# Gate products moved behind the first unit's transposes and first layer, expert 0's second-layer weights issued one step earlier, first rows rounded without a wait

## The reference

```python
def _moe_ref(x, w_in, w_out):
    h = x @ w_in
    g = h - np.tanh(h)
    return (g @ w_out).astype(np.float32)

def _moe2_ref(x, expert_emb, tau, w1, w2):          # x: 3072 x 384, 8 experts, width 1024
    xn = x / (np.linalg.norm(x, axis=-1, keepdims=True) + 1e-06)
    en = expert_emb / (np.linalg.norm(expert_emb, axis=-1, keepdims=True) + 1e-06)
    logits = xn @ en.T / tau
    expert_idx = np.argmax(logits, axis=1)
    logits_shift = logits - logits.max(-1, keepdims=True)
    probs = np.exp(logits_shift)
    probs /= probs.sum(-1, keepdims=True) + 1e-09
    gate_w = probs[np.arange(N), expert_idx]
    ...
    for e in range(E):
        mask = expert_idx == e
        ...
        h = np.maximum(x[mask] @ w1[e], 0.0)
        out[mask] = gate_w[mask, None] * (h @ w2[e])
```

## Time and profile before

| | |
|---|---|
| median of 3 runs | 851.17 us (847.74 to 852.49) |
| the profiled execution | 848.86 us, span 847.1 us |
| mean granted TensorE clock | 0.982 |
| TensorE busy | 819.8 us (97%) |
| VectorE, ScalarE, GpSimd busy | 640.3, 507.1, 217.9 us |
| moved by the transfers | 157.89 MB, mean 186 GB/s |

### The profile page before, as it was taken

One profiled execution on the slowest core, in us unless ns is written; L12 is line 12 of the kernel. 1 busy time (PEld: TensorE's weight loads), 2 busy tenths in 40 slices (PEclk: granted clock), 3 DMA queues, 4 the chain that ended last, 5 costly groups with the idle time before them and its releaser, 6 DMA issues. The chain is left out here.

```text
span 847.1 us, 18162 instructions
## 1 busy us (share of the span) xinstructions
PE 819.8 (97%) x5844; PEld 745.2 (88%) x5845; DVE 640.3 (76%) x983; ACT 507.1 (60%) x1057; POOL 217.9 (26%) x239
## 2 busy tenths in 40 slices
PE   8999989999999999999999999789999999999995
PEld 7767768889999999999999998689999999999994
DVE  8979959999998998998998997714546363637552
ACT  5756777767667667667667765215546363636552
POOL 6345524321111111111112331122222223132111
PEclk9999999999999999999999999769999999999998
DMA  9989943225234234224223755479696859693540
GB/s 245 279 255 278 297 131 94 66 80 179 100 106 154 87 109 151 99 87 161 101 100 123 235 188 182 172 244 387 240 332 238 292 203 388 245 362 121 176 160 9
DMA packets 86430, 157.89 MB, mean 186 GB/s; under 512 B 8060, under 2 KB 23566, under 8 KB 86385
## 3 DMA queue, kind: packets, MB, share of 16 engines
q1 hardware_dynamic: 58672, 100.82, 36.5%
q10 hardware_dynamic: 23744, 45.69, 15.0%
q0 software_dynamic: 3968, 10.82, 3.6%
HBM read 117.97 MB, written 40.70 MB: 187 GB/s over the span
## 5 line engine op out<-in xcount | busy, mean ns | idle before, releaser
L1303 POOL TENSOR_TENSOR ew_l<-ew_raw,ew_h 128x512 fp32r<-128x512 f32 x48 | 62.3, 1299 | 272.3 <-DVE poly L1521 268.0
L1227 PE MATMUL y_ps<-wout_h,g_h 128*128 128x392 f32 x384 | 130.8, 341 | 0.4 <-DVE g_l L1512 0.4
L1228 PE MATMUL y_ps<-wout_l,g_h 128*128 128x392 f32 x384 | 130.4, 340 | 0.0
L1229 PE MATMUL y_ps<-wout_h,g_l 128*128 128x392 f32 x384 | 130.3, 339 | 0.0
L1227 PE MATMUL h_ps<-xT_h,win 128*128 (+1 forms) x288 | 113.3, 394 | 1.2 <-DVE diff L1502 0.8
L1229 PE MATMUL h_ps<-xT_h,win 128*128 (+1 forms) x288 | 113.3, 394 | 0.0
L1228 PE MATMUL h_ps<-xT_l,win 128*128 (+1 forms) x288 | 112.8, 392 | 0.0
L1698 DVE SCALAR_TENSOR_TENSOR ex_hT_l<-e_bank,ex_hT_h 128x512 fp32r<-128x512 f32 x48 | 33.2, 691 | 102.8 <-ACT ex_hT_h L1952 88.0
L1853 PE MATMUL e_bank<-ex_xT_h,w_ex 128*128 128x256 f32 x288 | 81.8, 284 | 3.5 <-DVE ex_xT_l L1691 2.9
L1521 DVE COPY_PREDICATED poly<-large,diff 128x512 f32<-128x512 uint8 x96 | 72.0, 750 | 17.5 <-DVE poly L1517 17.5
L1854 PE MATMUL e_bank<-ex_xT_l,w_ex 128*128 128x256 f32 x288 | 81.5, 283 | 0.0
(11 more groups left out here) (244 smaller groups left out, 1994.0 us busy)
## 6 DMA issues: line engine op xcount, KB each, us to landing
w_raw<-in_w ACTq DMA_DIRECT2D x26, 1536.0 KB
ew_raw<-in_w SPq DMA_DIRECT2D x48, 256.0 KB, 2.7
w_h<-ew_h SPq DMA_DIRECT2D x48, 256.0 KB, 2.3
w_l<-ew_l SPq DMA_DIRECT2D x48, 256.0 KB, 2.0
w_ex<-w_h SPq DMA_DIRECT2D x8, 1536.0 KB
w_ex<-w_l SPq DMA_DIRECT2D x8, 1536.0 KB
kv_sb<-in_kv SPq DMA_DIRECT2D x24, 384.0 KB, 5.6
krT_sb<-in_krT SPq DMA_DIRECT2D x44, 192.0 KB, 6.1
```

The source lines that it names most:

```text
L1227: pe.matmul(out, lh, rh, start=start, stop=False)
L1228: pe.matmul(out, lh, rl, start=False, stop=False)
L1229: return pe.matmul(out, ll, rh, start=False, stop=stop)
L1303: pool.tensor_tensor(ew_l[:, slot, :], raw, ew_h[:, slot, :].bitcast(F32), ALU.subtract).then_inc(ew_l_made, 1)
```

## The change

Five edits, all at the boundary of the two blocks.

1. The buffer that holds the experts' weights is laid out anew (`unit_weights`, `second_weights`, `raw_at`; WIDE is 3072 values per partition). Both slots of second-layer weights now lie together at 2 to 6 WIDE, and the first-layer weights of odd units at 6 to 8 WIDE instead of 4 to 6. These odd weights no longer lie over the operands of the gate products; the second slot of second-layer weights does.
2. TensorE does both halves of the gate products in the expert block: the first twelve behind the transposes of unit 0, the other twelve behind the first layer of unit 0. The two pieces of filler behind the id products (10 and 3 turns) become one of 20 turns.
3. ScalarE's wait for `gates_turned` goes. It loads unit 1's weights and rounds unit 0's rows at once.
4. VectorE takes the gates behind the hidden rests of unit 0. TensorE's second tile of transposes for unit 1, which is written into the same bank as the gates, waits for that.
5. SyncE issues expert 0's second-layer weights inside the last step of the last group, ahead of the last piece's stores.

```diff
@@ -132,7 +132,7 @@
             w_at = nc.sbuf_base
             win = sbf("win", [P, 2, WIDE * PARTS], F32R)
             w_ex = nc.alloc_sbuf_tensor_at("w_ex", [P, SLOTS * 2 * PARTS * WIDE], F32R, offset=w_at)
-            raw_at = [w_at + 4 * (2 * PARTS * par + 1) * WIDE for par in range(2)] + [w_at + 4 * (SLOTS * 2 - 1) * PARTS * WIDE]
+            raw_at = [w_at + 4 * (6 * par + 1) * WIDE for par in range(2)] + [w_at + 4 * (SLOTS * 2 - 1) * PARTS * WIDE]
             w_raw = [nc.alloc_sbuf_tensor_at(f"w_raw{i}", [P, WIDE if i < 2 else PARTS * WIDE], F32, offset=at)
                      for i, at in enumerate(raw_at)]
             w_logit = sbf("w_logit", [P, KF, E])
@@ -172,14 +172,13 @@
 
 def unit_weights(w, par):
 
-    at = par * 2 * PARTS * WIDE
+    at = par * 6 * WIDE
     return w[:, at:at + WIDE], w[:, at + WIDE:at + 2 * WIDE]
 
 
 def second_weights(w):
 
-    slots = w[:, 0:2 * 2 * PARTS * WIDE].rearrange("p (s f) -> p s f", s=2)
-    return slots[:, :, 2 * WIDE:].rearrange("p s (h f) -> p s h f", h=2)
+    return w[:, 2 * WIDE:6 * WIDE].rearrange("p (s h f) -> p s h f", s=2, h=2)
 
 
 def load_second(eng, w, w2_h, w2_l, w_loaded, e):
@@ -1011,12 +1010,10 @@
                 pe.wait_ge(slot_hot, n // GROUP + 1)
                 last = pe.matmul(id_ps, oh_slot[:, n, :], rhs_id[:, n, :], start=(n == 0), stop=(n == NT - 1))
             last.then_inc(ids_turned, 1)
-            keep_warm(pe, h_ps[1], ident, 10)
-            pe.wait_ge(gates_placed, 2)
-            turn_gates(pe, 0)
-            keep_warm(pe, h_ps[1], ident, 3)
+            keep_warm(pe, h_ps[1], ident, 20)
 
         def turn_gates(pe, first):
+            pe.wait_ge(gates_placed, 2 * (first // PART + 1))
             for n in range(first, first + PART):
                 last = pe.matmul(gate_ps, oh_slot[:, n, :], rhs_gate[:, n, :, :].rearrange("p a s -> p (a s)"),
                                  start=(n == 0), stop=(n == NT - 1))
@@ -1257,6 +1254,12 @@
                         sp.wait_ge(xT_l_made, KD * g + KD)
                         load_group(sp, g + 1)
                     for f in range(KF):
+                        if last and f == KF - 1:
+                            sp.wait_ge(h_done, KF * CH)
+                            for i in range(MADE):
+                                sp.wait_ge(ew_h_stored[i], 16 * (NP // MADE + 2))
+                                sp.wait_ge(ew_l_stored[i], 16 * (NP // MADE + 2))
+                            load_second(sp, w, w2_h, w2_l, w_loaded, 0)
                         for j in pieces_at(g, last, f):
                             if is_first(g):
                                 sp.wait_ge(ew_l_made, j + 1)
@@ -1277,11 +1280,6 @@
                 for b in range(B):
                     sp.wait_ge(x_stored[b], 2 * 16 * (CH + 1))
                 groups(sp, group)
-                sp.wait_ge(h_done, KF * CH)
-                for i in range(MADE):
-                    sp.wait_ge(ew_h_stored[i], 16 * (NP // MADE + 2))
-                    sp.wait_ge(ew_l_stored[i], 16 * (NP // MADE + 2))
-                load_second(sp, w, w2_h, w2_l, w_loaded, 0)
                 store(CH - 1)
                 sp.wait_ge(x2_stored, 16 * NT)
                 for i in range(MADE):
@@ -1731,6 +1729,8 @@
 
                 def step(u, j, par, k):
                     hidden_low(u)
+                    if is_first(u):
+                        take_gates()
                     if k is not None:
                         solo_x_low(k)
                         weights_low(k, 0)
@@ -1750,7 +1750,6 @@
 
                 for t in range(2):
                     x_low(0, t)
-                take_gates()
                 steps(dve, step)
 
             @block.gpsimd
@@ -1835,6 +1834,8 @@
                 def transpose_tokens(u, j, par):
                     for t in range(2):
                         pe.wait_ge(gathered[2 * par + t], (j + 1) * 16)
+                        if t == 1 and isinstance(u, int) and u == 1:
+                            pe.wait_ge(gates_made, 1)
                         for a in range(KD):
                             last = pe.transpose(turn_bank(u, t)[:, a * P:(a + 1) * P], rows[:, 2 * par + t, a * P:(a + 1) * P],
                                                 ident[:, :])
@@ -1916,6 +1917,8 @@
 
                 def step(u, j, par, k):
                     first(u, par)
+                    if is_first(u):
+                        turn_gates(pe, NT // 2).then_inc(gates_turned, 1)
                     if k is not None:
                         transpose_solo(k)
                     second(u, 0, 0, KE)
@@ -1933,7 +1936,7 @@
 
                 pe.sem_inc(tile_done, 1)
                 transpose_tokens(0, 0, 0)
-                turn_gates(pe, NT // 2).then_inc(gates_turned, 1)
+                turn_gates(pe, 0)
                 steps(pe, step)
 
             @block.scalar
@@ -2032,7 +2035,6 @@
                         if not (isinstance(k, int) and k == NSOLO - 1):
                             load_solo(k + 1)
 
-                act.wait_ge(gates_turned, 1)
                 load_pair(1, 1)
                 for t in range(2):
                     x_high(0, t)
```

## The result

The changed kernel takes 852.59 us in the median of 20 runs (850.32 to 856.98), the kernel before 849.62 us in 20 runs beside it (846.77 to 854.27). The ratio is 1.0037, interval 1.0021 to 1.0052. The forecast was 843 us, between 838 and 848, so the prediction was wrong.

What follows compares the result with a forecast made beforehand. TensorE, busy 97% of the span, was taken as the bound, with time recoverable only where it idles or runs slowly. Terms -10.4 + 1.4 + 1.1 - 0.6 - 0.8 + 2.5 = -6.8 us gave 843 us, range 838 to 848.

Steps and rivals of the forecast that it cites:

- the one on expert 1's weights: Before unit 1's second layer: the later-issued transfer shares engines with ScalarE's loads, so TensorE stands; +2.5 us, between 0 and 6.
- The bad end of the term: Before unit 1's second layer: ScalarE's 4.7 MB go wholly ahead of expert 1's weights; 6 us of stall.
- The first layer's start: Unit 0's first layer, behind the barrier: starts at 549.3 instead of 559.74, 10.4 us earlier, between 9.6 and 10.7.
- The second gate products: Behind unit 0's first layer: the other twelve gate products stand uncovered; +1.4 us, between 1.4 and 2.77.
- the wait for `w_ready`: Before unit 0's second layer: SyncE passes expert 0's weights late, new TensorE idling; +1.1 us, between 0.9 and 1.5.
- The clock: First layer, whose first 3.6 us ran at 1.2 GHz: some speed comes back; -0.8 us, between -1.8 and +0.3.
- Full gain: Rival, 22%: the clock stays high and expert 1's weights are in time; -10.3 us, about 839.5.
- The routing is not shortened: Rival, 13%: first unit's weights still land late or filler outlasts VectorE; barrier at 549.6, sum -3.2 us, 847.
- Slower than before: Rival, 4%: transfers of the first two units starve, expert 1's weights hold TensorE over 13.5 us; 858.

Runs made afterwards that it cites:

- the fastest kernel: Against the kernel with 25 filler turns: SyncE passes expert 0's weights first and issues the first solo's load behind expert 1's; 840.26 us, ratio 0.9892.
- the 25 turns: 25 filler turns instead of 20, against the untied kernel with unit 1's first-layer weights issued in the routing; 841.62 us, ratio 0.9917.

## Why the prediction was wrong

**The step that failed is the one on expert 1's weights.** Its place was right, and it was named as the term that speaks against the change; its size was not. I took 21.5 us from issue to completion against a need of 19.3, so 2.5 us of stall. The need was exact: 19.3 us in the kernel without edit 5. The transfer took 26 to 27 us from issue to use in the four kernels that keep it tied to the gates beside the solo's load (26.2 after, 26.6 with expert 0 passed first, 27.1 without edit 5, 27.0 with the later gather). The shared rate was right too: from 572 to 592.6 us SyncE's queue moved 3.47 MB, 0.168 MB/us where I had 0.165. The two ends of the transfer were not. In the first 5.3 us the queue moved 0.08 MB, which loses 4.8 us; I had booked 2.5 us to the first bytes. And when expert 1's 3.15 MB were complete, the queue had moved 3.55 MB: bytes of expert 2's had gone ahead of the last ones of expert 1's, by the same rate some 2.4 us (an estimate), where I had rounded up by 0.2 for the slowest of the 16 engines. The 2.3 and the 2.4 us, less 0.3 for the rate, are the 4.4 between 21.5 and 25.9. The kernel without edit 5 agrees, with 0.23 MB in the first 6 us and 3.60 MB at the end. The bad end of the term, 6 us, had another reason, that ScalarE's 4.7 MB go wholly first; that did not happen, for ScalarE's queue reached 4.73 MB only when expert 1's weights were complete. In the profiled execution the stall was 5.28 us only because TensorE came 1.5 us late itself; in the kernels without that delay it was 7.7 to 8.8.

**The first layer's start: -8.0, not -10.4.** Of the missing 2.4 us, 1.0 is VectorE's remaining wait: I gave the first unit's weights 6 us to land as a lone transfer, and they took 8.4 from issue to use (11.0 before, 528.11 to 539.09, where the prediction's rival has 10.5). They were not alone: I had said of the stores behind expert 0's load that nobody waits for them, and SyncE's queue, with these stores, kept the engines until 533. Another 1.1 is the barrier. I put it 0.5 us behind VectorE, and it opened 1.6 us behind, held by GpSimd. The last 0.3 is between the barrier and the layer, where the twelve gate products ran at the low clock (2.75 us) and ended last; the prediction had priced that case but not taken it.

**The second gate products, 1.42 us, and the wait for `w_ready`, 1.28:** as predicted (1.4 and 1.1, within 0.9 to 1.5). Removing the second brought nothing, since the weights behind it were late.

**The clock: I booked -0.8 and it cost about 3.** The first layer from start to end took 9.86 us against 9.97, so nothing was won there. In the profiled execution the clock then stood at 0.51 in 569 to 572, 11 products where there would be 22, so 1.5 us; and at 0.50 behind the long idle time, about ten products at 0.32 instead of 0.17 us, 1.6 us. The second belongs to the stall: all five profiles of the changed kernel and its edits with an idle time of 4 us or more there show it. The first does not belong to the change: the four other kernels with the same 1.28 us idle time show a clock of 1.00 behind it (with the solo late, without edit 5, without the solo's 3 MB, with the later gather). It cost nothing in the end either: the weights were later still, and without it the stall would have been 6.8 us. The Trainium skill (TensorE: Matmul & The Clock Gate, Part 1: The HAM clock gate) says that the gate is set by how busy TensorE has been of late; for the idle times of 4 us and more the runs agree, for the one of 1.28 us they are divided. Nor is steady work a sure sign here: in the changed kernel the clock fell to 0.50 from 542 to 545 us, while TensorE ran filler without a break, and was back at 0.97 from 545 to 548. In the fastest kernel it stood at 0.53 from 551 to 554, in the first layer, with the 25 turns beside which it had stayed at 1.00.

**The rivals.** "Full gain" (22%) had no part in it. "The routing is not shortened" (13%) came true in part, and for its reason, stores that share the engines: 1.0 of VectorE's 3.6 us stayed. "Slower than before" (4%) meant over 855.4 us, with a stall of over 13.5 us. Nor did that come: 852.6 lies between it and the 846.9 below which the kernel would have been faster, a band that had 16% and in which the prediction looked only for gains. A stall of 9.3 us was needed to cancel the gains, because they were reckoned at their full size; 5.3 us did it, because the first layer's gain was 2.4 us smaller and the clock 3.9 us worse. Three misses of 2.4, 2.8 and 3.9 us, all in one direction, make 9.1 of the 9.4 us between -6.8 and +2.6 in the last row of the table. Behind the second and most of the third stands one cause, the transfer that came over 4 us later than I had it; stall and clock should have been one wide term rather than two narrow ones.

**The parts.** Edit 5 alone is -3.2 us, edits 1 to 4 alone are +7.8 (856.23 against 848.42), and together they are +3.0, which is their sum within the interval of the second; untying expert 1's load makes it -2.9, and putting both gate halves in front -4.9.

**What stays open.** Why SyncE's queue shows almost nothing for some 5 us behind an issue that falls beside ScalarE's; what decides whether the clock falls behind a short idle time or under filler; and why the barrier opens 2.6 to 2.8 us behind the end of GpSimd's second gather (2.69, 2.65, 2.69, 2.63 and 2.64 us in five kernels, at most 2.75 in five more). None of these was tried by itself.

## What to carry to other kernels

When work is moved behind a point, look at every transfer whose issue is tied to it, and at what the DMA engines do in the stretch that it leaves and in the one that it enters: here 3 MB left a stretch that then moved nothing and met 4.7 MB on another queue. Price such a transfer by its share of the rate, then add the slow start that the trace shows and the time that its last bytes lose when more is queued behind it, and count the clock lost behind a stall as part of the stall. A wait that is taken away ahead of a late transfer brings nothing; free the transfer first.

## What the runs showed of the hardware

- A queue whose transfer is issued beside another's shows little at first: 0.08 of 3.15 MB in 5.3 us, while the other moved 1.28; in the first 6 us of five other kernels it was 0.21 to 0.25 MB beside 1.42 to 1.47. From 575 to 578 us they share evenly, 0.55 MB each. The Trainium skill (DMA: Bandwidth & Descriptors, Queues, rings and completion order) has each engine alternate between its queues; that agrees with the even part and does not account for the start.
- Issuing is not free while earlier transfers are under way on the queue: the two transfers of a solo held ScalarE for 0.98 us (at 599 us, in the fastest kernel), 1.70 us in the changed kernel, and 5.26 us in the one with unit 1's weights early; it rounds nothing in that time.
- GpSimd's second gather of the first unit took 1.97 or 1.98 us where VectorE's subtraction of 128x1024 values had begun 0.07 to 0.08 us before it (eight kernels, before and after among them), and 0.95 us in four kernels where the two began within 0.01 us of each other.
